# A second token mixing that loads its input already turned, instead of turning it on TensorE

## The reference

```python
kv = k^T @ v per head; out = q @ kv                       # then RMS norm over the head, times a gain
x = out, tokens by channels                              # [8, 576, 512]
# first block (phase A below)
theta = x @ w_theta
y = w_tok_r @ (x * cos(theta)) + w_tok_i @ (x * sin(theta))      # mixes tokens
u = x + y
x2 = u + relu(u @ w_ch)                                   # mixes channels
# second block
h = relu(x2^T @ w_tok1) @ w_tok2                          # mixes tokens: 576 -> 256 -> 576   (phase B)
u2 = x2 + h^T
out = u2 + relu(u2 @ w_ch1) @ w_ch2                       # 512 -> 1536 -> 512                (phases C, D)
```

## Time and profile before

| | us |
|---|---|
| median of 3 runs | 1254.7 (1252.84 to 1254.87) |
| the profiled execution | 1253.56, span 1251.7 |
| PE busy in the span | 1208.0 (97%) |
| DVE, ACT, POOL busy | 796.4, 505.3, 365.3 |

### The profile page before, as it was taken

The page is one execution under the profiler, slowest core; times in us unless marked ns, Lnnn a source line. Parts: engine busy times, 40 slices in busy tenths (PEclk is TensorE's granted clock), DMA queues, the critical chain, the costliest instruction groups (busy, mean ns, idle before and its releaser), DMA issues.

```text
span 1251.7 us, 20559 instructions
## 1 busy us (share of the span) xinstructions
PE 1208.0 (97%) x7750; PEld 1170.9 (94%) x7750; DVE 796.4 (64%) x1204; ACT 505.3 (40%) x812; POOL 365.3 (29%) x216
## 2 busy tenths in 40 slices
PE   6989999999999999989999999999999889999998
PEld 5889999999899999979999999999999889999998
DVE  3875767566766667664455557677675676666664
ACT  3533324242524333242433345555565533333331
POOL 3453435444442534340462133133022320000000
PEclk9999999999999999989999999999999999999999
DMA  9922424242422420214546476857659999999972
GB/s 251 172 49 62 76 75 75 71 80 38 104 47 60 70 58 0 85 37 162 178 160 210 147 295 252 293 206 278 259 194 346 355 322 290 272 245 288 281 192 51
DMA packets 273422, 209.28 MB, mean 167 GB/s; under 512 B 196944, under 2 KB 244432, under 8 KB 272336
## 3 DMA queue, kind: packets, MB, share of 16 engines
q1 hardware_dynamic: 273360, 208.44, 56.6%
HBM read 127.40 MB, written 83.36 MB: 168 GB/s over the span
## 4 chain that ended last, share of the span: by engine, by line
PE 67%; issue 12%; DVE 7%; POOL 5%; DMA 3%; SPq 3%; ACT 2%; DVEq 0%; POOLq 0%; ACTq 0%
PE bank L42 12%; PE bank L44 12%; PE bank L43 12%; PE bank L1165 9%; PE bank L1167 9%; PE bank L1166 9%; PE bank L236 2%; DVE weights_fraction L605 1%; POOL z_z L770 1%; PE bank L918 1%; SPq L149 1%; DVE tokens_cos L602 1%; DMA weights_down<-w_scratch 1%; PE bank L224 1%; DMA weights_raw_u<-u_scratch 1%
## 5 line engine op out<-in xcount | busy, mean ns | idle before, releaser
L42 PE MATMUL bank<-weights_tok,z_z 128*128 128x288 f32 x576 | 175.0, 304 | 14.6 <-ACT z_z L455 9.2
L43 PE MATMUL bank<-weights_tok,z_z 128*128 128x288 f32 x576 | 170.7, 296 | 0.0
L44 PE MATMUL bank<-weights_tok,z_z 128*128 128x288 f32 x576 | 170.6, 296 | 0.0
L42 PEld LDWEIGHTS bank<-weights_tok,z_z 128*128 128x128 f32 x576 | 109.2, 190 | 18.1 <-ACT z_z L455 10.6
L43 PEld LDWEIGHTS bank<-weights_tok,z_z 128*128 128x128 f32 x576 | 109.3, 190 | 0.0
L44 PEld LDWEIGHTS bank<-weights_tok,z_z 128*128 128x128 f32 x576 | 109.0, 189 | 0.0
L755 POOL TENSOR_TENSOR weights_rms_inverse<-weights_mean_squares,weights_minus_half 128x8 f32<-128x8 f32 x40 | 65.5, 1637 | 137.3 <-DVE weights_mean_squares L572 137.2
L770 POOL TENSOR_TENSOR z_z<-tokens_cos,z_z 128x512 fp32r<-128x512 f32 x32 | 51.7, 1617 | 177.5 <-ACT z_z L455 176.6
L462 ACT ACTIVATE weights_x_channel_major<-attention_u 128x288 fp32r<-128x288 f32 x64 | 28.4, 444 | 149.7 <-DVE attention_u L633 149.7
L42 PE MATMUL bank<-weights_x_channel_major,weights_ch 128*128 128x288 f32 x256 | 77.5, 303 | 0.0
L43 PE MATMUL bank<-weights_x_channel_major,weights_ch 128*128 128x288 f32 x256 | 75.4, 294 | 0.0
(11 more groups left out here) (271 smaller groups left out, 3747.3 us busy)
## 6 DMA issues: line engine op xcount, KB each, us to landing
g_scratch<-attention_staged SPq DMA_DIRECT2D x36, 960.0 KB, 4.6
weights_g<-g_scratch SPq DMA_DIRECT2D x24, 1152.0 KB, 8.4
g_scratch<-attention_staged SPq DMA_DIRECT2D x36, 384.0 KB, 4.7
x_scratch<-attention_u SPq DMA_DIRECT2D x8, 1152.0 KB, 4.2
u_scratch<-attention_u SPq DMA_DIRECT2D x8, 1152.0 KB, 6.1
weights_raw_u<-u_scratch SPq DMA_DIRECT2D x6, 1536.0 KB, 8.8
qkv_u_left<-u_scratch SPq DMA_DIRECT2D x12, 768.0 KB, 7.4
qkv_k<-in_k_dram SPq DMA_DIRECT2D x32, 256.0 KB, 4.8
```

Source lines behind the costliest of these rows:

```text
L42: eng.matmul(out, w[0], x[0], start=first, stop=False)
L43: eng.matmul(out, w[0], x[1], start=False, stop=False)
L44: return eng.matmul(out, w[1], x[0], start=False, stop=last)
```

## The change

Phase A makes a second copy of x2 in DRAM, token-major (`x2t_dram`, [8, 576, 512]). When the channel groups of a quarter of the channels are complete, DVE turns it in 32x32 blocks (`turn_x2`) into a tile that shares bytes with the upper tiles of `z`, and SP stores it in four DMAs per quarter (`store_turned`), sixteen per batch, each of 32 partitions and 18 blocks, in pieces of 128 bytes. ACT waits for all of them in the next batch before `z_hi` of tile 2.

Phase B loads the tokens (`load_tokens`: three DMAs with pieces of 2 KB) into one buffer (`raw_x`; the first batch has one of its own, `raw_first`) and splits them from there in three pieces of 2, 2 and 1 tiles. The PE transposes and their banks are gone; the mixing has six banks and does six groups with the first half of the hidden units, then the same six with the second, then two more. `hidden` counts its pieces (`p_x`), so that ACT may overwrite a piece of the split tokens while PE is at the next. The order on SP, ACT and DVE changes as the diff shows.

```diff
@@ phase_a, sync
             sp.dma_start(x2_dram[n, :, :, :], u[:, :, :]).then_inc(s_store, DMA)
+            for c in range(NC):
+                store_turned(n, c)
+        def store_turned(n, c):
+            sp.wait_ge(d_turned, NC * n + c + 1)
+            for part in range(PARTS):
+                first = c * P + part * SIDE
+                sp.dma_start(x2t_dram[n, :, first:first + SIDE].rearrange("(b s) d -> s b d", s=SIDE),
+                             turned[c // 2][part * SIDE:(part + 1) * SIDE, c % 2, :].rearrange("p (b d) -> p b d", d=SIDE)
+                             ).then_inc(s_turned, DMA)
@@ phase_a, tensor
-                if not more and g >= 3:
-                    nxt["transpose"](pe, 0, 0, g - 3)
@@ phase_a, scalar
+            if j == 2:
+                wait(act, s_turned, PARTS * NC * DMA * b)
             act.wait_ge(d_z, 2 * (NT * b + j + 1))
@@ phase_a, vector
+        def turn_x2(b, c):
+            dve.wait_ge(d_x2, NG * b + NC + c + 1)
+            if c == 0:
+                wait(dve, s_turned, PARTS * NC * DMA * b)
+                dve.wait_ge(g_zlo, NK * (b + 1))
+                dve.wait_ge(p_tok, NG * (b + 1))
+            dve.transpose(turned[c // 2][:, c % 2, :], u[:, c, :]).then_inc(d_turned, 1)
...
                 relu_add(b, g)
+                if g > NC:
+                    turn_x2(b, g - NC - 1)
...
-                if not more and g >= 4:
-                    nxt["x_lo"](dve, 0, 0, g - 4)
+                if not more and g >= 5:
+                    nxt["x_lo"](dve, 0, g - 5)
             if more:
                 for j in range(1, NT):
                     x_lo(b + 1, j)
-            else:
-                nxt["x_lo"](dve, 0, 0, NT - 1)
+            turn_x2(b, NC - 1)
@@ phase_b
+    ps_h, ps_y = banks[3:5], [banks[i] for i in (7, 1, 0, 2, 5, 6)]
+    PIECES = [(0, 2), (2, NJ), (NJ, NT)]
...
+    def load_tokens(sp, n):
+        raw = raw_first if n == 0 else raw_x
+        if n == 1:
+            sp.wait_ge(d_tok, len(tok_weights))
+        elif n > 1:
+            sp.wait_ge(d_xlo, NPX * n)
+        sp.dma_start(raw[:, 0:NJ, :], x2t_dram[n, 0:NJ * P, :].rearrange("(j p) d -> p j d", p=P)).then_inc(s_tokens, DMA)
+        for first in (0, LEFT):
+            sp.dma_start(raw[first:first + LEFT, NJ, :], x2t_dram[n, NJ * P:S, :]).then_inc(s_tokens, DMA)
...
     def load_second(sp):
+        sp.wait_ge(*prev["p_theta"])
+        sp.wait_ge(*prev["turned_but_last"])
+        load_tokens(sp, 0)
         load(sp, 1, 1)
...
         load_quarter(sp, 1, 0)
         load_quarter(sp, 1, 1)
+        load_tokens(sp, 1)
         for n in range(B):
             if n + 2 < B:
                 if n + 3 == B:
                     sp.wait_ge(*prev["stored"])
                 load(sp, n % 2, n + 2)
+                if n + 3 == B:
+                    sp.wait_ge(*prev["turned"])
+                load_tokens(sp, n + 2)
             sp.wait_ge(d_u, NG * (n + 1))
             sp.dma_start(u2_dram[:, :, n * S:(n + 1) * S], u2[:, :, :]).then_inc(s_st, DMA)
@@ phase_b, tensor
-                pe.wait_ge(d_hlo, NM * (n - 1) + mt + 1)
...
+                pe.wait_ge(d_hlo, NM * n)
+            part(0, 0, False)
+            part(0, 1, True)
+            part(1, 0, False)
+            part(2, 0, False).then_inc(p_h, 1)
+            part(1, 1, True)
+            part(2, 1, True)
...
+        def body(n):
+            mix(n)
+            hidden(n + 1)
@@ phase_b, scalar
+    def x_hi(act, n, piece):
+        first, end = PIECES[piece]
+        raw = raw_first if n == 0 else raw_x
+        act.wait_ge(s_tokens, 3 * DMA * (n + 1))
+        wait(act, p_x, NPX * (n - 1) + piece + 1)
+        act.activation(xtm[0][:, first:end, :], raw[:, first:end, :], ACT.Copy).then_inc(a_xhi, 1)
...
-        for mt in range(NM):
-            hidden_hi(0, 0, mt)
-        act.wait_ge(*prev["d_x2"])
+        act.wait_ge(*prev["turned"])
...
             if n + 1 < B:
-                for j in range(NT):
-                    x_hi(act, *after(i, pair), j)
+                x_hi(act, n + 1, 0)
+            for mt in range(NM):
+                hidden_hi(n, mt)
+            for piece in range(1, NPX):
+                if n + 1 < B:
+                    x_hi(act, n + 1, piece)
@@ phase_b, vector
         def batch(n, i, pair, more=True):
             if more:
+                x_lo(dve, n + 1, 0)
+            for mt in range(NM):
+                hidden_lo(n, mt)
+            if more:
+                for piece in range(1, NPX):
+                    x_lo(dve, n + 1, piece)
             for g in range(NG):
+                residual(n, i, pair, g)
@@ phase_c, tensor
             if n == 0:
                 pe.wait_ge(a_hi, 1)
-                for b in (bank_b(0), bank_b(1), bank_c):
+                pe.wait_ge(*prev["d_u_but_two"])
+                for b in (bank_b(0), bank_b(1), bank_c, bank_f):
                     open_bank(b)
```

More of the change, by code:

```diff
@@ L547, in body @@
                 act.wait_ge(d_z, 2 * NT * B)
-                for j in range(NT):
-                    nxt["x_hi"](act, 0, 0, j)
+                for piece in range(3):
+                    nxt["x_hi"](act, 0, piece)
         body(0, first=True)
@@ L955, in mix_first @@
                     mix_part(g, mt)
[L957 to L960 removed]
+            for g in range(NY, NG):
+                pe.wait_ge(d_u, NG * n + g - NY + 1)
+                for mt in range(NM):
+                    mix_part(g, mt)
         pe.wait_ge(d_tok, len(tok_weights))
[L963 to L977 removed]
@@ L1123, in gpsimd @@
         gp.wait_ge(s_up[2], DMA)
+        gp.wait_ge(*prev["turned"])
         add(up_sum, a11, a21, ALU.subtract)
```

186 lines of the change are left out of this document (79 added, 107 removed).

## The result

| | before | after |
|---|---|---|
| median us | 1254.7 (1252.8 to 1254.9) | 1305.7 (1303.4 to 1309.0), four runs each |
| ratio | | 1.041, 95% interval 1.039 to 1.044 |
| profiled execution, its span | 1253.6, 1251.7 | 1303.4, 1301.6 |
| last residual of phase B's first batch (T0) | 603.2 | 621.0 |
| last residual of its eighth batch (T7) | 707.5 | 760.5 |

The change makes the kernel 4.1% slower: 51 us where 34 were forecast, half as much again. The median lies at the very end of the range of 1272 to 1306: one of the four runs is above it (1309.0), and so is the time that the ratio gives, 1.0412 x 1254.7 = 1306.4.

The account below looks back on a forecast made before the run. PE, busy 97% of the span, was taken to bound the kernel. 15.7 + 12.4 - 2.2 + 10.2 = +36.1 us on 1253.6 gave 1289.7, stated as 1289, range 1272 to 1306.

Parts of the forecast that it names:

- Phase A, cost 0: Phase A: DVE's turns, SP's turned stores and ACT's wait for them are all covered by existing idle time; cost 0.
- Step 1: Step from phase A to B: batch 1's tokens land late, so batch 0's last residual ends at 618.9, not 603.2; +15.7 us.
- (a): Step from phase A to B: ACT now waits until all turned stores have landed; no separate size given.
- Step 2: Phase B, batches 1 to 6: late tokens hold PE's next operand on ACT; period 17.0 us for 14.93, +12.4 us.
- Step 3: Phase B's batch 7: no tokens behind it, so it takes 12.74 us; -2.2 us.
- Step 4: PE's clock halves after idling, once at the step to phase B and in five of six batches; +10.2 us.
- Phases C and D: Phases C and D: operations and loads hang on phase B's last residual and u2 store as before; cost 0, no recovery.
- rival 1: Phase B: tokens come late, but PE's clock holds or loads flow faster; +21, 1275 us; chance 0.10.
- rival 2: Phase A stalls as well, z_hi(b,2) on ACT waiting for the turned stores; 1322 us; chance 0.07.
- rival 3: Phase B gains the whole 15.3 us, tokens landing within 2.6 us of the last residual; 1238 us; chance 0.04.
- rival 4: Transposes gone, but phase B's batches break even and the step to phase B is hidden; 1254 us; chance 0.02.

Follow-up runs that it names:

- phase_a_alone: Kernel before plus only phase A's half (turns, turned stores, ACT's wait) for batches 0 to 6, second copy unread: 1253.5 us, ratio 1.0009.
- seam: Kernel after, with batch 1's tokens loaded ahead of phase A's last x2 store and turned stores, and ACT's first split ahead of its wait for them: 1299.5 us.
- u2_late: Kernel after, with SP issuing the u2 store of batch n only once the tokens of batch n+2 have landed: 1305.5 us.
- filler: Kernel after, with 20 useless matmuls of 512 columns on PE between hidden(n+1) and mix(n+1): 1307.7 us.
- no_left: Kernel after without the two narrow token loads from batch 2 on, part of the computation left out: 1301.1 us.
- half_behind: Kernel after, with the second half of the x2 load issued behind the tokens instead of ahead of them: 1299.1 us.
- pieces_8k: Kernel after, with the large token load of batches 2 to 7 in pieces of 8 KB instead of 2 KB, changing the token order: 1307.1 us.
- all_pieces_turned: all_pieces, with the first two quarters' turned stores in phase A's last batch issued ahead of the x2 store: 1253.1 us, ratio 0.9989 to before.
- all_pieces: tokens_first_up plus seam, with tokens loaded in three pieces, each with its own semaphore and issued when its buffer piece is free: 1251.8 us, ratio 0.9986 to before.
- tokens_first: Kernel after, with SP issuing the tokens of batch n+2 ahead of the x2 load: 1269.7 us, ratio 1.011.
- tokens_first_up: tokens_first, with ACT's third weight split moved from phase B's second batch to its first: 1265.8 us, ratio 1.012 to before.

## Why the prediction was right and where it was wrong

**Phase A, cost 0: right.** phase_a_alone measures it. A turned store took 0.67 us to issue, forecast 0.61; a turn 0.76, forecast 0.85.

**Step 1, +15.7: right.** T0 moved by 17.8 us, the forecast with its fall of the clock being 17.4. Counted from the last x2 store, which comes 1.2 us earlier in after, it is 19.0. The terms hold one by one (issue of the tokens at 598.5, forecast 599.5; x_hi at 608.3, forecast 608.7); 2.88 MB at 410 GB/s are 7.0 us and not 7.2. seam shows that it was SP's order, as argued, and also what the prediction had named as (a) and not priced: behind the tokens stands the wait for the turned stores, worth some 8 us by itself.

**Step 2, +12.4: the mechanism right, its main term too small.** The six periods grew by 34.9 us where steps 2 and 4 gave 20.9. The periods of 17 to 19 us that the prediction asked for came out at 20.5 to 22.2. The failed step is L, the time from the last residual to the landed tokens. "3.8 us for the x2 half, 1.31 MB more at 410 GB/s is 3.2" counts queued bytes and lets everything else overlap. Measured were 9.07 us in place of 6.8, six times 2.27 = 13.6 us, and the runs name the parts: the store behind the tokens in the queue (0.8, which I had at zero), the two narrow loads (1.1, where their bytes gave 0.6), and the half and the large load together (0.4 + 6.6 + 0.1 = 7.1, where I had 6.2 without the narrow ones). The check against before's 7.1 us for 1.9 MB should have warned: there the last transfer was a store that nothing had to follow. The upper end of L, 7.5, was too low too; the time came to the end of the range and not far beyond it only because the range also held seven falls of the clock at 2.6 us each and 3 us for which the prediction gives no source. That is luck.

The Trainium skill ("DMA: Bandwidth & Descriptors", section "Two DMAs through the same engine are not ordered") says that the descriptors of a queue start in order but are pipelined. By that a transfer behind can delay one ahead; u2_late agrees, with its 0.8 us. The formula that the prediction cites from the same page of the Trainium skill would have been farther off: the estimate of 6.4 us stands against 9.07.

**Step 3, -2.2: wrong.** T6 to T7 is 13.54 us, but before it was 13.26 and not 14.93: in the last batch before had no transposes either. The saving was counted where there was nothing to save. One of before's other periods was 16.20, which I had not read. The two errors are +2.5 and -1.3 us. The seventh set of turns lies ahead of T0, in the first batch.

**Step 4, +10.2: right in kind, a little low.** The clock fell at the step and in six batches, not five; PE idled 6.1 to 6.5 us in each and not 4.2. By the windows the clock cost 2.8 us at the step and, as what is left of the six periods after 9.07, 3.06 and 7.02 us, 11.0 in the batches (half of PE's work at the low clock gives 11.6), 13.8 in all. filler shows the term by removing it from four periods.

**Phases C and D, 0: right, though the table has -3.1.** Their program is the same in all kernels here but for one bank that before opens later, and from T7 to the end of the span it takes 544.2 us in before, 541.1 in after, 543.3 in phase_a_alone, and between 540.8 (no_left) and 544.3 (filler) in the others, whatever was changed. Part of it is the clock: before has a fall at 733.8 behind its wait for the first load of u2, which costs it 1.7 us; seam, half_behind, pieces_8k and all_pieces_turned have it too (543.5 to 543.7), and after does not. It is not all: filler and phase_a_alone have no such fall. Windows of after at the same wait:

```profile
783.50:785.50 2.00, 0.24 (x2) 0.00 (x0) 0.70 (x1) 1.57 (x3) 0.00 (x0) 1.00 1.04 428
785.50:789.00 3.50, 3.42 (x18) 3.12 (x19) 2.50 (x5) 1.82 (x6) 3.16 (x2) 1.00 0.74 305
```

PE idles for 1.8 us and the clock stays at 1.00 behind it. So -3.1 lies within what executions of the same phases differ by, and no run shows an effect of the change in it; single runs of this kernel should not be read closer than that.

**The rivals.** Rivals 1 to 4 did not occur. What rival 3 asked for, tokens issued earlier and there within 2.6 us of the last residual, is what all_pieces does (2.3 us): its 12.74 us periods came in four of seven, and 7.9 us at the step to phase B and 4.0 in the one long period kept its 1238 away.

## What to carry to other kernels

When a transfer is put in the place of an engine's work, write down for it the last event that it waits for, what is queued ahead of it and behind it, and every instruction queued behind its first user. Here tokens whose buffer had been free for 6.7 us (last x_lo at 635.5, last residual at 642.2) stood behind a load that waited for the last residual, and on ACT and DVE PE's next operand stood behind them; moving two lines on SP took back 36 of 51 us. Price a transfer on a path by one of its size measured from issue to use, narrow companions included, and not by its bytes.

## What the runs showed of the hardware that I had not expected

- DVE's subtraction of two tiles in SBUF (128x1024) takes 1.23 us alone. In tokens_first it took 3.63 us, and ended 1.1 us behind POOL's elementwise instruction (641.5 to 644.9) that had started first; the POOL instruction started next took 4.43 us in place of 3.5. In tokens_first_up the two started together (624.4): DVE took its 1.23 us and POOL 4.59. So here the one that came later waited until the other was through, and the one in possession lost nothing. Before, DVE read these tiles from banks, and a POOL instruction beside it kept its 3.5 us. The Trainium skill ("Trainium Architecture — The Big Picture", section "What this means for kernel authors") says that DVE and GpSimd share a port pair under an exclusive lock; the trace agrees.
- ACT stood 2.2 to 3.9 us at one place of 13 kernels, and went on 1.5 to 1.7 us behind the start of an 8 KB packet of an instruction queue. The profile's list of waits names no releaser for it; the list of DMA queues has the packet.
- A 1.05 MB load lands 5.2 us after its issue with nothing near it, and 0.8 us later for a store issued behind it in the same queue.
- Stores of 576 pieces of 128 bytes take SP 0.52 us each to issue in a long row, but two or three near its start 1.0 to 2.1; at the step to phase B sixteen of them are 10.7 to 11.9 us of SP's time in one row and 13.3 in two.
- The time lost to a fall of the clock did not shrink with the idle time ahead of it: with tokens landing 1.1 us earlier (no_left) PE got back 0.6 us a batch, since it then worked more of the stretch at 1.2 GHz (4.7 to 5.3 us in place of 3.0 to 4.2, and 6.1 in the sixth).
